# Idle-time matmuls in the attention prologue of a fused linear-attention and feed-forward kernel

## What is computed

```
for t in range(S):                                  # attention, per batch and head
    m_new = max(f_gate + m, i_gate)
    C = exp(f_gate + m - m_new) * C + exp(i_gate - m_new) * outer(v, k)
    n = exp(f_gate + m - m_new) * n + exp(i_gate - m_new) * k
    y = sigmoid(o) * (C @ q) / max(abs(n @ q), 1)
h = x @ w_in;  x = (h * sigmoid(1.702 * h)) @ w_out  # feed-forward
out = sum over e of p[e] * (relu(x @ w1[e]) @ w2[e]) # four experts
```

## Time and profile before

| what | us |
|---|---|
| median of 3 runs | 681.08 |
| lowest and highest | 677.59, 683.44 |
| profiled execution, its own time | 677.59 |
| its span in the profile | 675.8 |

### The profile page before, as it was taken

How to read it: one execution, slowest core, us unless ns; L and a number is a source line. 1 busy time by engine, 2 the same in 40 slices (tenths; PEclk the granted TensorE clock), 3 DMA queues, 4 the chain that set the end, 5 groups by cost and what they waited for, 6 DMA issues and landing times.

```text
span 675.8 us, 9643 instructions
## 1 busy us (share of the span) xinstructions
PE 637.0 (94%) x3628; PEld 561.5 (83%) x3628; DVE 346.1 (51%) x577; ACT 192.8 (29%) x366; POOL 158.3 (23%) x85
## 2 busy tenths in 40 slices
PE   1888699999999999998999999999999999999998
PEld 0666588889788897787889999889988889999888
DVE  4698577766776675566633333333323333333333
ACT  4444354452554434322311111121102121111110
POOL 0565332330233121366702202222040000000000
PEclk9999999999999999999999999999999999999999
DMA  6863712305133000121201110111110000000012
GB/s 157 269 196 118 179 35 58 84 1 132 49 88 88 0 0 17 49 116 66 97 1 48 40 48 1 39 48 40 48 41 1 1 1 1 0 1 1 1 39 79
DMA packets 9621, 38.47 MB, mean 57 GB/s; under 512 B 1144, under 2 KB 3416, under 8 KB 8144
## 3 DMA queue, kind: packets, MB, share of 16 engines
q1 hardware_dynamic: 9584, 37.94, 18.9%
HBM read 35.78 MB, written 2.16 MB: 56 GB/s over the span
## 4 chain that ended last, share of the span: by engine, by line
PE 84%; DVE 10%; ACT 2%; issue 2%; DMA 2%; SPq 0%; ACTq 0%; DVEq 0%
PE bank L420 12%; PE bank L422 12%; PE bank L421 12%; PE bank L411 9%; PE bank L412 9%; PE bank L413 9%; PE bank L408 5%; PE bank L409 5%; PE bank L380 2%; DVE g_lo L219 2%; DVE state_lo L686 2%; PE bank L357 2%; DVE floor L693 1%; DVE gbuf L719 1%; PE bank L349 1%
## 5 line engine op out<-in xcount | busy, mean ns | idle before, releaser
L420 PE MATMUL bank<-dn_hi,g_lo 128*128 128x320 f32 x576 | 180.3, 313 | 5.3 <-DVE ysum L727 3.8
L422 PE MATMUL bank<-dn_hi,g_hi 128*128 128x320 f32 x576 | 178.0, 309 | 0.0
L421 PE MATMUL bank<-dn_lo,g_hi 128*128 128x320 f32 x576 | 177.9, 309 | 0.0
L631 ACT ACTIVATE g_hi<-bank 128x512 fp32r<-128x512 f32 x96 | 57.4, 598 | 273.5 <-PE bank L413 273.5
L805 DVE SCALAR_TENSOR_TENSOR g_lo<-bank,g_hi 128x512 fp32r<-128x512 f32 x96 | 66.3, 692 | 120.0 <-ACT g_hi L631 119.8
L420 PEld LDWEIGHTS bank<-dn_hi,g_lo 128*128 128x128 f32 x576 | 108.2, 188 | 8.9 <-DVE ysum L727 4.6
L411 PE MATMUL bank<-xT,up_hi 128*128 128x512 f32 (+1 forms) x288 | 113.1, 393 | 0.0
L412 PE MATMUL bank<-xT,up_lo 128*128 128x512 f32 (+1 forms) x288 | 113.0, 392 | 0.0
L413 PE MATMUL bank<-xT,up_hi 128*128 128x512 f32 (+1 forms) x288 | 113.0, 392 | 0.0
L421 PEld LDWEIGHTS bank<-dn_lo,g_hi 128*128 128x128 f32 x576 | 108.2, 188 | 1.1
L422 PEld LDWEIGHTS bank<-dn_hi,g_hi 128*128 128x128 f32 x576 | 108.1, 188 | 0.0
(11 more groups left out here) (122 smaller groups left out, 700.3 us busy)
## 6 DMA issues: line engine op xcount, KB each, us to landing
raw<-qk_d SPq DMA_DIRECT2D x12, 960.0 KB, 7.3
up_raw<-up_d SPq DMA_DIRECT2D x12, 768.0 KB, 5.1
dn_raw<-down_d SPq DMA_DIRECT2D x12, 640.0 KB, 4.1
kvo<-kvo_d SPq DMA_DIRECT2D x12, 488.0 KB, 3.5
out_d<-acc SPq DMA_DIRECT2D x2, 640.0 KB, 3.3
out_d<-acc SPq DMA_DIRECT2D x4, 160.0 KB, 1.8
scratch_d<-split SPq DMA_DIRECT2D x1, 192.0 KB, 6.9
consts<-consts_d SPq DMA_DIRECT2D x1, 145.0 KB, 2.2
```

Source lines behind the costliest of these rows:

```text
L420: mm(dst[:, 0:DM], g_lo[:, par, f, toks], dn_hi[s][:, f, :], start=f == 0, stop=False)
L421: mm(dst[:, 0:DM], g_hi[:, par, f, toks], dn_lo[s][:, f, :], start=False, stop=False)
L422: last = mm(dst[:, 0:DM], g_hi[:, par, f, toks], dn_hi[s][:, f, :], start=False, stop=f == NF - 1)
L631: go(g_hi[:, j % 2, f, :], UPB[f][:, :], ACT.Relu).then_inc(hi2_done, 1)
```

## The change

Calls of keep_warm are added around the attention that stands alone, all into DNB[1]: eleven matmuls ahead of its first slot, two behind every stage of it that PE has a part in (seven such stages for each of four units, so 28 pairs or 56 matmuls), and five behind its last slot. These are 72 matmuls of 128x512 in bf16. No wait, buffer, DMA or instruction of another engine is added, removed or moved.

```diff
         pe.wait_ge(gates_copied, 2)
         pe.wait_ge(const_set, 5)
 
+        keep_warm(DNB[1], 11)
         for slot in range(ALONE_SLOTS):
             for uq, stage in att_stages(slot, ALONE, ALONE_PITCH):
                 attention(uq, uq, 0, stage, uq > 0, True)
+                if stage in (SCORE0, SCORE1, INTER, STATE, FINISH, STACK, TRANSPOSE):
+                    keep_warm(DNB[1], 2)
+        keep_warm(DNB[1], 5)
 
         with pe.Fori(0, NG - 1) as g:
             ffn_group(g, True)
```

## The result

The changed kernel takes 687.62 us (median of 4 runs, 687.50 to 688.89), against 680.58 us before in the same comparison: 7.0 us more, and 0.6 us outside the range that was given. The record holds 19 further executions of it, and all 23 together run from 685.99 to 694.27 us with a median of 689.40. The ratio of 1.0138, 95% interval 1.0096 to 1.0179, goes by all 23 (their mean is 689.9 us), so the loss is between 7.0 and 9.4 us. The span of the profiled execution is 690.6 us, longer than the 685.6 to 687.1 of the four.

What follows compares the result with a forecast made beforehand. PE was taken to bound the kernel, though POOL and DVE mostly set the attention stretch's period. Gains of 1.25 (first unit), 1.0 (periods), 0.4 (last transposes) and 2.7 (feed-forward start) sum to 5.35 us, giving 675.7 us, range 672 to 687.

Steps and rivals of the forecast that it cites:

- the first one of the sum: Attention alone: 2.4 GHz reached during the eleven or the first unit's first matmuls, then kept; added matmuls cost 0.217 us each.
- the case in which the pairs hold it: Attention alone: level up for good from the first unit on, total gain 5.35 us, chance 0.5.
- the level stays low, and PE becomes the bound: Attention alone at 1.2 GHz: PE needs 18.4 us per period against 14.5; +13 to +15.5 us, about 695, chance 0.13.
- up and down: Attention alone: idle time at 2.4 GHz loses the level, so low and high alternate; 677 to 687 us, chance 0.15.
- The eleven at no cost: Ahead of the first scores: the wait for the exponents covers the eleven, 4.7 us at 1.2 GHz, so cost nothing.
- First unit -1.25 us: First scores to end of second L350: 4.94 us becomes 3.69 at 2.4 GHz with two pairs in between.
- the late rise: First unit begins low and pays +1.7 us, 678.7 in all; chance 0.22, shared with only the feed-forward start gained.
- Periods -0.33 us each: Periods two to four: PE's chain piece of 1.78 us becomes 1.45 with one pair, three times, 1.0 us together.
- the sum of 1.01 + 0.43 us: Second scores to ACT's xT copy, per period: PE's piece at 2.4 GHz plus one pair, 1.45 us instead of 1.78.
- The tail at no cost: Last transposes to first L408: seven matmuls, 1.5 us, just fit 1.49 us of idle; 1.5 us late if level low.
- Feed-forward start -2.7 us: First group, first L408 to first attention piece: 10.15 us becomes 7.47 at 2.4 GHz, the largest gain.

Runs made afterwards that it cites:

- The fours: Changed kernel with four instead of two matmuls behind every stage, eleven and five kept: 687.55 us against 679.81 before, ratio 1.0115.
- the clear chain: Changed kernel with 33 ahead and four behind stages, none behind second scores or the first unit's first scores and INTER: 685.45 us against 680.55, ratio 0.9980.
- the last one: Changed kernel with 28 ahead, one or four behind stages off the chain, twelve ahead of the last transposes: 674.33 us against 682.68, ratio 0.9897.

## Why the prediction was wrong

The step that failed is the first one of the sum: "My likeliest case is that the level rises during the eleven or in the first unit's first matmuls and then stays up, so I sum at 2.4 GHz". It rose during the eleven, at 13.7 us, and did not stay: not through the 5.7 us of idle time behind them, and not through the pairs. With two dense matmuls behind each stage PE was busy for 27.47 of 30.6 us in the change, and for all of 25.98 us in the pairs alone, at 1.2 GHz. I had noted that 60 us of busy PE had not earned the higher level. I still gave a chance of one half to the case in which the pairs hold it, with no row in which a mixture like theirs had done so.

What came is mostly the rival "the level stays low, and PE becomes the bound", given 0.13, with a piece of the one called up and down, given 0.15. The latter's sign is there: matmul lengths change back and forth, and in the one high piece PE idles, busy for 7.24 of 10.0 us, before the level falls. The price was that of the low case, and about right. PE's need at the low level was put at 18.4 us a period and measured at 17.89. The rival's +14 us were for a stretch wholly low; with 10.2 us high it was +10.8. The point from which it decides, a little over half of the stretch at the low level, was passed with 62 of 72 us.

Point by point:

- The eleven at no cost: right (ratio 0.9999 alone). The rule cited against them was right too. The Trainium skill ("TensorE: Matmul & The Clock Gate", Part 1) says that an idle stretch between bursts brings the half rate back; the trace agrees, the level fell at 17.1 us, 2.6 us after the end of the eleven.
- First unit -1.25 us: not in the change, where the second L350 ended 6.6 us after the first L349 instead of 4.94, the +1.7 of the late rise. At the high level and without pairs its basis held: 2.82 us measured.
- Periods -0.33 us each: the sum of 1.01 + 0.43 us was never reached in the change. The fours show the mechanism at work (1.88 us with four in between), the clear chain its size (13.78 us).
- The tail at no cost: it was not free. At 1.2 GHz the seven took 2.69 us, and the first L408 started 92.24 - 89.03 = 3.21 us after the transposes did, where it was 2.36: 0.85 us late, against the 1.5 given for that level.
- Feed-forward start -2.7 us: right, 7.54 in place of 10.15 us, the one gain that the change has.
- The range missed the median of the four by 0.6 us and that of all 23 by 2.4 us. It ended where the up and down case ended, at 687, and left out the low case whole; what came lies between the two. That the miss is so small is luck of the mixture, since the likeliest case had the sign wrong.

The forecast of what a held level is worth was right, then, as far as the other kernels show it part by part; whether it would be held was not for the rows of before to say. It took a denser and differently placed filling to hold it.

Why two behind each stage don't hold the level and four mostly do stays open. The filling was not varied finely enough to say what the clock gate weighs, and the two kernels with fours ahead of the last one, with mean granted clocks from 0.985 down to 0.958 and from 0.997 down to 0.958, show that the same program can hold it in one execution and lose it in the next.

## What to carry to other kernels

Matmuls issued only to hold the clock are free where PE idles, and cost their whole length where they stand on the chain, at either level. While the level is low that length is double, and in a stretch with 2 us of room per 14.5 us they turned PE into the bound. So count them at the low level, place none on the chain, and take the level from matmul durations where the clock column has nothing on record. The part next to dense work is the safe one: here it gave 0.4% alone and 0.5% when moved into PE's idle time, where the whole lost 1.0 to 1.4%.

## What the runs showed of the hardware

Being busy is not what earned the clock: PE stayed at 1.2 GHz while busy for 32.64 of 34.0 us in the change and for 25.98 of 25.98 us in the pairs alone. The page's clock column counts a stretch before the first recorded change as full speed; the same work reads 1.00 before and 0.50 in the eleven alone.

The scatter of this kernel is partly the clock too. Of the 18 runs of before taken beside the last comparison, the six with a mean granted clock of 1.000 took 678.4 to 679.9 us, the two at 0.997 took 681.2 and 681.6, and the ten at 0.993 to 0.995 took 682.5 to 685.4. In the 32 of the comparison before it the classes overlap: thirteen at 1.000 took 677.1 to 681.9 us, twelve at 0.997 took 679.9 to 682.0, seven below took 683.1 to 684.6. The traces show these dips as 3.4 us at 1.2 GHz, none in the profiled execution of before, one or two in the third group of the others. By an estimate from these rows a clock halved for 3.4 us costs 1.7 us at most, and the third group grows by 2 to 3 us with each dip, so the dip is not the whole price. In the third group they come during or up to 1.5 us behind idle times of PE of 1.8 to 3.7 us, which end with DVE's ysum; other such idle times have no dip behind them. What makes those waits differ from run to run was not tried.

The Trainium skill ("SBUF — State Buffer", Who interferes with whom) says that an instruction of the vector engine with two inputs in SBUF contends with one of GpSimd that reads SBUF, for a pair of ports that works as an exclusive lock. The traces agree. In the changed kernel, one row of POOL and two of DVE:

```profile
...
48.06 3.43 POOL L830 TENSOR_TENSOR up_lo<-up_raw,up_hi 128x1536 fp32r<-128x1536 f32 x1 [10.00 <-ACT up_hi L604]
...
48.73 3.13 DVE L690 TENSOR_TENSOR state_lo<-state,state_hi 40x336 fp32r<-40x336 f32 x1 [0.55 <-ACT state_hi L548]
...
152.97 0.49 DVE L690 TENSOR_TENSOR state_lo<-state,state_hi 40x336 fp32r<-40x336 f32 x1
...
```

Beside up_lo, which runs from 48.06 to 51.49, state_lo takes 3.13 us and ends at 51.86; at 152.97, with no POOL operation beside it, the same operation takes 0.49 us. This is what keeps the level's worth in this stretch small: state_lo and floor, 3.28 and 2.37 us of the fours' period at 2.4 GHz, do not shrink with TensorE's clock.
